# A gated unit on one core: chunks 2 to 7 as seven products of sums of quarters

## The reference

```
x: 1152 tokens x 512
gate = 1 / (1 + exp(-(x @ w_gate)))      # w_gate, w_val: 512 x 1536
val  = x @ w_val
x    = (gate * val) @ w_out              # w_out: 1536 x 512
```

## Times and profile before

| | us |
|---|---|
| median of 3 runs | 1251.75 (1251.71 to 1252.18) |
| the profiled execution, whole | 1252.13 |
| its span | 1250.3 |
| PE busy | 1241.0 |
| DVE busy | 750.6 |
| ACT busy | 585.2 |
| POOL busy | 576.0 |

### The profile page before, as it was taken

The page is one execution under the profiler, slowest core; times in us unless marked ns, Lnnn a source line. Parts: engine busy times, 40 slices in busy tenths (PEclk is TensorE's granted clock), DMA queues, the critical chain, the costliest instruction groups (busy, mean ns, idle before and its releaser), DMA issues.

```text
span 1250.3 us, 19809 instructions
## 1 busy us (share of the span) xinstructions
PE 1241.0 (99%) x7546; PEld 1139.2 (91%) x7546; DVE 750.6 (60%) x1622; ACT 585.2 (47%) x1235; POOL 576.0 (46%) x466
## 2 busy tenths in 40 slices
PE   8999999999999999999999999999999999999999
PEld 7888888899999899998998998998998998998998
DVE  7999999862223134767566466466466466466444
ACT  7999999843333244444353233233233233233221
POOL 6577777722212365754255255255255255255221
PEclk9999999999999999999999999999999999999999
DMA  6667677421110332122122122122122122122112
GB/s 171 119 120 118 120 119 119 78 60 51 34 50 26 95 99 60 56 68 81 54 77 72 53 76 75 53 76 75 53 78 73 53 77 75 52 78 73 51 35 93
DMA packets 98905, 95.29 MB, mean 76 GB/s; under 512 B 14528, under 2 KB 73152, under 8 KB 98816
## 3 DMA queue, kind: packets, MB, share of 16 engines
q1 hardware_dynamic: 98496, 93.77, 30.2%
q10 hardware_dynamic: 320, 0.33, 0.1%
HBM read 88.59 MB, written 2.40 MB: 73 GB/s over the span
## 4 chain that ended last, share of the span: by engine, by line
PE 93%; ACT 5%; DVE 1%; issue 0%; DMA 0%; ACTq 0%; POOL 0%; POOLq 0%
PE bank L1100 12%; PE bank L1102 12%; PE bank L1101 11%; PE bank L1255 11%; PE bank L1256 11%; PE bank L1257 10%; PE bank L965 4%; PE bank L1048 4%; PE bank L1047 4%; PE bank L1049 4%; PE bank L938 4%; PE bank L978 3%; PE bank L979 3%; ACT probs L1364 2%; ACT pT_hi L1283 2%; DVE part_min L1640 1%
## 5 line engine op out<-in xcount | busy, mean ns | idle before, releaser
L1763 DVE TENSOR_TENSOR c<-bank,c 128x256 f32<-128x256 f32 (+1 forms) x448 | 197.2, 456 | 280.6 <-PE bank L1102 274.0
L896 POOL TENSOR_TENSOR w_lo<-w_raw,w_hi 128x512 fp32r<-128x512 f32 x128 | 163.8, 1300 | 287.6 <-ACT w_hi L1283 287.6
L1256 PE MATMUL bank<-w_lo,h_hi 128*128 128x512 f32 x578 | 225.2, 390 | 0.0
L1255 PE MATMUL bank<-w_hi,h_hi 128*128 128x512 f32 x578 | 225.1, 389 | 0.0
L1257 PE MATMUL bank<-w_hi,h_lo 128*128 128x512 f32 x578 | 224.4, 388 | 0.0
L1484 ACT ACTIVATE h_hi<-c 128x256 fp32r<-128x256 f32 (+1 forms) x256 | 112.6, 445 | 160.4 <-DVE c L1763 160.1
L1257 PEld LDWEIGHTS bank<-w_hi,h_lo 128*128 128x128 f32 x578 | 108.6, 188 | 22.9
L1255 PEld LDWEIGHTS bank<-w_hi,h_hi 128*128 128x128 f32 x578 | 108.6, 188 | 20.8
L1256 PEld LDWEIGHTS bank<-w_lo,h_hi 128*128 128x128 f32 x578 | 108.7, 188 | 20.0
L1640 DVE TENSOR_REDUCE part_min<-bank 128x1 f32<-128x256 f32 (+2 forms) x216 | 114.7, 558 | 20.1 <-PE bank L979 13.6
L1283 ACT ACTIVATE c<-bank 128x256 f32<-128x256 f32 (+1 forms) x64 | 26.2, 410 | 214.2 <-PE bank L1102 214.2
(11 more groups left out here) (153 smaller groups left out, 2994.3 us busy)
## 6 DMA issues: line engine op xcount, KB each, us to landing
w_raw<-in_moe_w SPq DMA_DIRECT2D x64, 512.0 KB, 3.5
w_raw<-in_moe_w SPq DMA_DIRECT2D x64, 256.0 KB, 3.1
q_raw<-in_q SPq DMA_DIRECT2D x30, 288.0 KB, 4.7
k_raw<-in_k SPq DMA_DIRECT2D x30, 288.0 KB, 7.9
wo_raw<-in_moe_w_out SPq DMA_DIRECT2D x16, 384.0 KB, 3.4
v_raw<-in_v SPq DMA_DIRECT2D x16, 288.0 KB, 5.0
gv_raw<-in_moe_w_gate SPq DMA_DIRECT2D x12, 256.0 KB, 3.0
gv_raw<-in_moe_w_val SPq DMA_DIRECT2D x12, 256.0 KB, 3.2
```

The lines of the kernel that those rows point to most:

```text
L896: ins = nc.gpsimd.tensor_tensor(w2_lo[:, u % 2, c], w2_raw[:, c], f32(w2_hi[:, u % 2, c]), ALU.subtract)
L1255: nc.tensor.matmul(dst, hh, wh, start=(first and c == 0), stop=False)
L1256: nc.tensor.matmul(dst, hh, wl, start=False, stop=False)
L1763: nc.vector.tensor_tensor(dst[:, 0:w], bank[:, (u + b) % 3, 0:w], other[:, 0:w], ALU.add).then_inc(done, 1)
```

## The change

Chunks 0, 1 and 8 to 11 stay as they are (`CONV`; the loop is unrolled). Chunks 2 to 7 (`SEVEN`) are made as 12 units u: chunk f = 2 + u // 2, token set n = u % 2 (0: 2 x 256 tokens, 1: 2 x 320). In a unit, x is cut in four quarters (first or second half of its 512 columns, first or second run of tokens) and the weights in four (upper or lower 256 rows; gate or value). Seven products of 6 matmuls give what eight give today; S1, S2 and S3 use quarters of x, the others sums of them. Set 0 uses banks 0 to 2, set 1 banks 3 to 5.

- The token sums (`xs`) are made once, while chunks 0 and 1 run: x_hi + x_lo by VectorE for set 0 (`sx_first`) and GpSimd for set 1 (`sx_second`), four chained subtractions for each set on VectorE (`st_sums`), split by ScalarE (`st_hi_part`) and GpSimd (`st_lo_part`, two operations of 1024 and two of 1280 columns). They lie in unused parts of h1.
- The weight sums of each chunk: two on GpSimd (`sw_sums_13`), two on VectorE (`sw_sums_24`), 256 columns each, then split: ScalarE `sw_hi_raw` (512 and 256 columns) and `sw_hi_sums` (1024), GpSimd `sw_lo_raw` (512 and 256) and `sw_lo_sums` (2 x 512), into a ring of two.
- After the products, VectorE adds them up (`x_and_y`, `gates`, `gated`), ScalarE takes both sigmoids at once, VectorE multiplies SBUF by SBUF, ScalarE copies to h1_hi (`sh_hi_part`) and GpSimd subtracts for h1_lo (`sh_lo_part`, 512 or 640 columns).
- `sbuf_op` is a scalar_tensor_tensor that multiplies by 1.0 first.
- TensorE's order in a unit is S1, S6, S5, then S7 and S4 of the unit before, then S2, S3. The last unit's S7 and S4 come behind the first gate product of chunk 8.
- SyncE no longer waits for x_tail ahead of the loads of chunk 2 and on, and wo_raw's first load moves behind the last S4.

The core of the diff (left out: allocations, semaphores, the hand-over to chunk 8, and GpSimd's and ScalarE's parts that the list above describes in full):

```diff
+SEVEN = range(2, 8)
+CONV = (0, 1, 8, 9, 10, 11)
+SEVEN_UNITS = 2 * len(SEVEN)
+ST_ORDER = ((0, 1), (0, 0), (1, 1), (1, 0))
+CONV_STEPS = len(CONV) * NBLK
...
+            def seven_product(u, b, tile, x):
+                f, n = seven(u)
+                for c in range(2):
+                    mm = split_product(bank[:, 3 * n + b, 0:WIDE[n]], sw_hi[f % 2][:, tile + c], sw_lo[f % 2][:, tile + c],
+                                       x(0, c), x(1, c), c == 0, c == 1)
+                return mm
...
+            def seven_bank_free(u, b, done, conv_done):
+                if u >= 2:
+                    pe.wait_ge(done, u - 1)
+                else:
+                    pe.wait_ge(conv_done, conv_step(1, b) + 1)
+            def seven_165(u):
+                f, n = seven(u)
+                conv_done = (sig_done, h32_done)[n]
+                if n == 0:
+                    pe.wait_ge(sw_split, 3 * sw_count(f) + 3)
+                seven_bank_free(u, 0, value0_done, conv_done)
+                seven_product(u, 0, 0, seven_quarter(u, 0, 0)).then_inc(s1_ready, 1)
+                if u < 2:
+                    pe.wait_ge(st_lo_done, 2 * u + 1)
+                seven_bank_free(u, 1, s7_added, conv_done)
+                seven_product(u, 1, 8, seven_sum(u, 1, 1)).then_inc(s6_ready, 1)
+                if u < 2:
+                    pe.wait_ge(st_lo_done, 2 * u + 2)
+                seven_bank_free(u, 2, gate1_done, conv_done)
+                seven_product(u, 2, 6, seven_sum(u, 0, 0)).then_inc(s5_ready, 1)
+            def seven_74(u):
+                pe.wait_ge(sX_done, u + 1)
+                seven_product(u, 1, 10, seven_sum(u, 0, 1)).then_inc(s7_ready, 1)
+                pe.wait_ge(gate0_done, u + 1)
+                seven_product(u, 0, 4, seven_sum(u, 1, 0)).then_inc(s4_ready, 1)
+            def seven_23(u):
+                pe.wait_ge(s1_copied, u + 1)
+                seven_product(u, 0, 2, seven_quarter(u, 1, 0)).then_inc(s2_ready, 1)
+                pe.wait_ge(sY_done, u + 1)
+                seven_product(u, 2, 12, seven_quarter(u, 1, 1)).then_inc(s3_ready, 1)
...
+            for u in range(SEVEN_UNITS):
+                seven_165(u)
+                if u >= 1:
+                    seven_74(u - 1)
+                seven_23(u)
...
+            def sx_second():
+                pool.wait_ge(x_done, LAST // 2)
+                pool.wait_ge(x_tail, NHEAD - LAST)
+                for k in range(2):
+                    nc.gpsimd.tensor_tensor(xs[1][:, :, k * WIDE[1]:(k + 1) * WIDE[1]], f32(sx_part(x_hi, 1, k)),
+                                            f32(sx_part(x_lo, 1, k)), ALU.add).then_inc(sx_made[1], 1)
...
+            def sw_sums_13(f):
+                raw, to = gv_raw[f % 2], sw_sums(f)
+                pool.wait_ge(gv_loaded[f % 2], 32 * (f // 2) + 32)
+                if f == SEVEN[0]:
+                    pool.wait_ge(x_done, LAST // 2)
+                    pool.wait_ge(x_tail, NHEAD - LAST)
+                elif f == SEVEN[1]:
+                    pool.wait_ge(v_ready, conv_step(0, NBLK - 1) + 1)
+                else:
+                    pool.wait_ge(sw_split, 3 * sw_count(f))
+                nc.gpsimd.tensor_tensor(to[:, 0], raw[:, 1, 0:2], raw[:, 1, 2:4], ALU.add).then_inc(sw_summed13, 1)
+                nc.gpsimd.tensor_tensor(to[:, 2], raw[:, 0, 0:2], raw[:, 1, 0:2], ALU.subtract).then_inc(sw_summed13, 1)
...
+            sw_sums_13(SEVEN[0])
+            sx_second()
+            sw_lo_raw(SEVEN[0])
+            sw_lo_sums(SEVEN[0])
+            for nth, (n, j) in enumerate(ST_ORDER):
+                st_lo_part(n, j, nth)
+            for u in range(SEVEN_UNITS):
+                f, n = seven(u)
+                if n == 0 and f + 1 in SEVEN:
+                    sw_sums_13(f + 1)
+                    sw_lo_raw(f + 1)
+                elif f + 1 in SEVEN:
+                    sw_lo_sums(f + 1)
+                elif n == 0:
+                    gv_lo_part(f + 1, (f + 1) % 2)
+                if u >= 1:
+                    sh_lo_part(u - 1)
+            sh_lo_part(SEVEN_UNITS - 1)
...
+            def st_hi_part(n, j):
+                at = (slice(None), slice(2 * j, 2 * j + 2))
+                act.wait_ge(st_summed, 4 * n + 4)
+                copy(st_hi(n)[at], xs[n][at]).then_inc(st_hi_done, 1)
+            def sw_hi_raw(f):
+                hi, raw = sw_hi[f % 2], gv_raw[f % 2]
+                gv_there(f)
+                if sw_count(f) >= 2:
+                    act.wait_ge(s4_ready, 2 * sw_count(f) - 2)
+                copy(hi[:, 0:4], raw[:, 0]).then_inc(sw_hi_done, 1)
+                copy(hi[:, 4:6], raw[:, 1, 2:4]).then_inc(sw_hi_done, 1)
+            def sw_hi_sums(f):
+                act.wait_ge(sw_summed13, 2 * sw_count(f) + 2)
+                act.wait_ge(sw_summed24, 2 * sw_count(f) + 2)
+                copy(sw_hi[f % 2][:, 6:14], sw_sums(f)[:].rearrange("p s c n -> p (s c) n")).then_inc(sw_hi_done, 1)
+            def s1_copy(u):
+                n = u % 2
+                act.wait_ge(s1_ready, u + 1)
+                if u >= 2:
+                    act.wait_ge(gated_done, u - 1)
+                elif u == 1:
+                    act.wait_ge(h1_lo_done, conv_step(1, 2) + 1)
+                copy(sg[n][:, 0:WIDE[n]], bank[:, 3 * n, 0:WIDE[n]]).then_inc(s1_copied, 1)
+            def gates(u):
+                n = u % 2
+                act.wait_ge(gate0_done, u + 1)
+                act.wait_ge(gate1_done, u + 1)
+                nc.scalar.activation(sg[n][:], sg[n][:], ACT.Sigmoid).then_inc(gates_done, 1)
...
+            act.wait_ge(x_done, LAST // 2)
+            act.wait_ge(x_tail, NHEAD - LAST)
+            for u, (f, blk) in enumerate(FIRST_F1):
+                sigmoid_part(u, blk)
+                h1_hi_part(f, u, blk)
+                if u == 1:
+                    sw_hi_raw(SEVEN[0])
+                    sw_hi_sums(SEVEN[0])
+                if u in (2, 3):
+                    for n, j in ST_ORDER:
+                        if n == u - 2:
+                            st_hi_part(n, j)
+            for u in range(SEVEN_UNITS):
+                f, n = seven(u)
+                s1_copy(u)
+                if u >= 1:
+                    gates(u - 1)
+                if f + 1 in SEVEN:
+                    if n == 0:
+                        sw_hi_raw(f + 1)
+                    else:
+                        sw_hi_sums(f + 1)
+                elif n == 0:
+                    gv_hi_part(f + 1)
+                if u >= 1:
+                    sh_hi_part(u - 1)
+            gates(SEVEN_UNITS - 1)
+            sh_hi_part(SEVEN_UNITS - 1)
...
+            def sbuf_op(dst, a, b, op):
+                return nc.vector.scalar_tensor_tensor(dst, a, 1.0, b, ALU.mult, op)
+            def sx_first():
+                dve.wait_ge(x_done, LAST // 2)
+                dve.wait_ge(x_tail, NHEAD - LAST)
+                for k in range(2):
+                    sbuf_op(xs[0][:, :, k * WIDE[0]:(k + 1) * WIDE[0]], f32(sx_part(x_hi, 0, k)), f32(sx_part(x_lo, 0, k)),
+                            ALU.add).then_inc(sx_made[0], 1)
+            def st_sums(n):
+                w, x = WIDE[n], xs[n]
+                x11, x12 = x[:, 0:2, 0:w], x[:, 0:2, w:2 * w]
+                x21, x22 = x[:, 2:4, 0:w], x[:, 2:4, w:2 * w]
+                dve.wait_ge(sx_made[n], 2)
+                sbuf_op(x11, x12, x11, ALU.subtract).then_inc(st_summed, 1)
+                dve.wait_ge(st_summed, 4 * n + 1)
+                sbuf_op(x12, x22, x12, ALU.subtract).then_inc(st_summed, 1)
+                dve.wait_ge(st_summed, 4 * n + 2)
+                sbuf_op(x22, x22, x11, ALU.subtract).then_inc(st_summed, 1)
+                dve.wait_ge(st_summed, 4 * n + 3)
+                sbuf_op(x21, x21, x22, ALU.subtract).then_inc(st_summed, 1)
+            def sw_sums_24(f):
+                raw, to, n = gv_raw[f % 2], sw_sums(f), 2 * sw_count(f)
+                dve.wait_ge(gv_loaded[f % 2], 32 * (f // 2) + 32)
+                dve.wait_ge(sw_summed13, n + 1)
+                sbuf_op(to[:, 1], to[:, 0], raw[:, 0, 0:2], ALU.subtract).then_inc(sw_summed24, 1)
+                dve.wait_ge(sw_summed24, n + 1)
+                sbuf_op(to[:, 3], raw[:, 0, 2:4], to[:, 1], ALU.subtract).then_inc(sw_summed24, 1)
...
+            def add(dst, u, b, other, done):
+                n = u % 2
+                nc.vector.tensor_tensor(dst, bank[:, 3 * n + b, 0:WIDE[n]], other, ALU.add).then_inc(done, 1)
+            def x_and_y(u):
+                n = u % 2
+                dve.wait_ge(s6_ready, u + 1)
+                dve.wait_ge(s1_copied, u + 1)
+                if u >= 2:
+                    dve.wait_ge(sh_lo_done, u - 1)
+                add(half(cv, n, 0), u, 1, half(sg, n, 0), sX_done)
+                dve.wait_ge(s5_ready, u + 1)
+                dve.wait_ge(sX_done, u + 1)
+                add(half(cv, n, 1), u, 2, half(cv, n, 0), sY_done)
+            def gates(u):
+                n = u % 2
```

(43 more changed lines are left out.)

259 lines of the change are left out of this document (183 added, 76 removed).

## The result

The changed kernel takes 1266.76 us (median of 4 runs, 1266.25 to 1267.66), the kernel before 1251.73 us beside it (4 runs): 1.012 times as long (95% interval 1.0103 to 1.0138), 15.0 us more. The forecast was 1262, in the range 1246 to 1268. The profiled execution took 1266.72 us with a span of 1264.9, 14.6 more than the span before. The profiled executions come to the end of the last x_lo at different times, 267.3 to 270.3 us, though nothing ahead of it was changed. So I also give the time of the stage itself, from there to the start of the last gate or value matmul: 147.0 us before, 161.8 in the changed kernel.

What follows compares the result with a forecast made beforehand. The prediction took TensorE's matmuls, in flight for 99% of the span at full clock, as the bound. Its terms -9.0 + 13.8 + 2.3 + 3.0 = +10.1 us on the 1251.75 us median gave 1262, range 1246 to 1268.

Steps and rivals of the forecast that it cites:

- TensorE's share: Chunks 2 to 7: 504 narrower matmuls take 66.9 us in place of 75.9, -9.0 us if TensorE never waits.
- The table load: Before the first sigmoid: the load waits for x_tail, TensorE starts at 270.15, +2.6 us, swallowed by what follows.
- The start: Chunks 0 and 1 to unit 0's end: sums and h1_lo held on the SBUF read path, +13.8 us.
- The wait of 3.2 us at (1,1): Chunks 0 and 1: TensorE, done with the gate half at 285.0, stands until h32 of step 2 at 288.2.
- the 13 us of waits: Sign to look for: TensorE's waits between 268 and 306 us total 13 us, or 3 if rival 1 is right.
- Chunk 3: The later chunks' walk, begun at 306.1 us, gives 314.2 against 311.95: +2.3 us.
- Each later chunk: Chunks 4 to 7: weights split at T+11.85, TensorE done at T+11.15; 0.7 us waiting a chunk, +3.0 in all.
- the walk: Step-by-step timing of a later chunk: VectorE's product takes the read path at T+4.6, GpSimd starts at T+5.3.
- rival 3: Chunk loop worse than walked: product and sums each held, 2 us more a chunk, +8, 1267; 0.20 with rival 4.
- Rival 4: TensorE's clock falls in the gaps of the start: +4 to +6 us, 1267; chance 0.20 together with rival 3.
- Sum: Whole kernel: -9.0 + 13.8 + 2.3 + 3.0 = +10.1 us, giving 1262.
- Rival 1: The SBUF read path hardly matters: start +2.8, later chunks 0, so 1245.8 us, faster; chance 0.20.

Runs made afterwards that it cites:

- e4: Changed kernel with VectorE's gating product cut to 16 columns and its weight sums of chunks 4 to 7 to 8 of 128 columns: 1255.97 us.
- e13: e12 with ScalarE's waits for x_done and x_tail behind the first sigmoid, no early small sigmoid, one st_lo ahead of the last h1_lo: 1248.93 us.
- e2: Changed kernel with a one-column sigmoid on ScalarE ahead of the wait for x_tail, so the table loads early: 1268.77 us.
- e12: e11 with the gating product in a buffer of its own per token set and VectorE's two weight sums behind that product: 1252.21 us.
- e1: Changed kernel with its new VectorE operations of two SBUF inputs written as plain two-tensor operations, not the scalar form: 1267.35 us.
- e7: Changed kernel with the sigmoid of chunks 2 to 7 written to PSUM, so the gating product has one input there: 1263.18 us.
- e3: Changed kernel with GpSimd's two sx_second operations writing a constant and reading nothing (set 1's token sums left out): 1262.85 us.
- e11: e10 plus e2's early table load and a reordered start, with sx_second and st_lo on VectorE between the steps: 1258.15 us.
- e5: Changed kernel with ScalarE's copy of tiles 0 to 3 of the next weights waiting for product 2, not product 4: 1266.24 us.
- e10: Changed kernel with e7 and e5 together, and VectorE's two weight sums and ScalarE's copy of the sums moved ahead: 1263.64 us.
- e6: Changed kernel with 18 filler transposes on TensorE ahead of its wait for the split weights at chunks 4 to 7: 1267.23 us.

## Why the prediction was right, and where its sizes were off

The range held, and so did the direction. The mechanism was right: two engines that both read SBUF take turns, and this loses more than the matmuls save; the clock, which the forecast left at full, adds 3.0 us. In the sizes two errors offset each other in part, so that 1262 is off by 4.8 us and not by 7 is luck.

- *TensorE's share, -9.0.* Right in its rate: in e4 and e13 341 matmuls fit in 45 us, 0.132 us each, as (0.1189 + 0.1466) / 2 says.
- *The table load.* Forecast 268.3 and TensorE at 270.15; measured 268.13 and 270.06. "Swallowed by what follows": yes, e2 took it away for nothing. What was left of the first sigmoid's wait was worth 0.5 us of the stage even with the sums out of the way (e12 to e13).
- *The start, +13.8.* The steps as forecast and measured: h1_lo(0) done 276.0 and 275.7; h32 of step 1 at 279.3 to 279.9 and 278.7; of step 2 at 287.6 and 285.7; of step 3 at 297.0 and 294.7. Unit 1's S1 started at 303.80, 11.5 us later than the 292.3 that before's order allows. Mechanism right, 2.3 too much: the alternation costs VectorE less per turn than I took. The wait of 3.2 us at (1,1) didn't appear in the trace because the slow matmuls had filled it; in e1, at full clock, 1.2 of it did. So of the 13 us of waits that were to show between 268 and 306 us, 6.7 stand in the trace.
- *Chunk 3, +2.3.* From unit 1's S1 to chunk 3's it is 7.78 us, where full pace needs 5.83: +2.0.
- *Each later chunk, 0.7 us, +3.0.* This is the term that was mis-sized. The starts of S1 in chunks 3 to 7 are 311.58, 323.56, 337.47, 350.96 and 364.85: 11.98, 13.91, 13.49, 13.89 us in place of 11.9 each, +8.7 against 11.15, and 1.6 more in the last chunk. It has three parts. In chunk 3, where the product is first at the read path as the walk assumed, the walk is right: weights split after 11.93 us, forecast 11.85. In chunks 4 and 6 GpSimd is first by 0.16 us and the product and the second sum are held: 1.9 us more each, 3.8 in all. That is rival 3's mechanism and its size, 2 us a chunk, in every second chunk. The walk took the order of the two for granted and left out that x_and_y waits for GpSimd's h1_lo, which puts VectorE later in a chunk that TensorE enters without a wait (the first addition comes 2.8 us after S1 in chunk 4, 1.7 in chunk 3). This order of the two is read from the trace; no run changed it alone. And in chunks 5 and 7 the clock fell: 1.5 us each, 3.0 in all.
- *Rival 4, the clock.* It fell, as I had not counted, but it cost nothing where I had priced it. In the start TensorE had to wait anyway: from the restart behind h32 of step 3 to unit 1's S1 it is 8.50 us with the lower clock from 294.1 to 300.9 us (changed kernel), and the same with it from 294.9 to 298.3 (e1). In the chunk loop, where I had no fall, two of them cost 3.0 of the 14.6 us, and a third one in e1 cost 1.5 more. They follow TensorE's waits for the weights; in e4, e7 and e12, where those are shorter or gone, the clock stays full in the loop.
- *Sum.* -9.0 + 11.5 + 2.0 + 8.7 + 1.6 = +14.8, measured +14.6 in the span. 2.6 too much in the start and chunk 3 and 7.3 too little in the later chunks made the 4.8 us by which 1262 is short.

Rival 1, that the read path hardly matters, is shown false by e3 (writing instead of reading) and e7 (PSUM instead of SBUF). What stays open is how the 5.5 us of e11 divide between holds, order and clock, since that run changed all three; how e12's gain divides between the buffer and the sums; and the 1.1 us that go with the tile `early`.

## What to carry to other kernels

Before work is given to VectorE and GpSimd "in parallel", see whether VectorE's has two inputs in SBUF and GpSimd's reads SBUF: then add their times, and give the work to the engine that is shorter in it, or let one operand come from PSUM. When a loop is slower than every engine's own work in it, follow one buffer around: who writes it, who reads it, and which in-order engine waits for the last reader with other work behind it. Taking one hold away moves the wait to the next (e5, e7, e10 gave 0.5, 3.6 and 3.1 us, most of it the clock's; e12 on top of them all the rest): judge such an edit by the loop's period, and not by the wait that went. And a filler that is to keep an engine busy must end before what it waits for is there: look whether its last instruction stands behind that moment, or the test measures the filler (e6).

## What the hardware showed that I had not expected

- An operation that comes 0.3 us after GpSimd's waits for it in full, 2.9 us (e2), and again for the next: the turn is a whole instruction, not a part.
- After a wait of 2.5 us the granted clock sometimes fell (changed kernel, e3: 0.57 in 270 to 274) and sometimes didn't (e1: 1.00 from 270 to 276), though the programs differ in one instruction's form only, or in one operation; after the 3.8 us at 291 to 298 it fell in each of them that had that wait (e1: 0.61 in 294 to 298; e10: 0.50 in 296 to 300). At the start of chunk 3, 1.8 us of waiting were followed by a fall in e1 and by none in the changed kernel.
- One fall costs 1.5 us where TensorE's product 4 releases the next weights (chunk 3 in e1 against the changed kernel), and nothing where TensorE waits for VectorE's and ScalarE's row anyway (8.50 us with a long fall and with a short one).
- 0.3 us in the order of two operations of different engines go with 1.9 us a chunk: the product 0.12 us ahead of GpSimd's operation or 0.16 us behind it.
